# Attention scores of the next tile moved to the end of a step, and one weight buffer shifted by 64 bytes

## The chip, the cores and the metric

The kernel runs on one core of a Trainium2 chip. The metric is the device time of one execution in microseconds, the median of several runs; lower is better.

## The reference

Three computations follow each other. The first is a gated linear-attention recurrence (an mLSTM cell) over 2 batches, 8 heads, 768 time steps and head dimension 40. Its result, 1536 tokens of 320 numbers, goes through an RMS norm and a gated feed-forward layer of width 1536, and then through a second one of width 2048:

```
m' = max(f + m, i);  C = exp(f+m-m')*C + exp(i-m')*outer(v, k);  n = exp(f+m-m')*n + exp(i-m')*k
y  = sigmoid(o) * (C @ q) / max(|n . q|, 1)            # for each head and time step
xn = x / rms(x) * rms_g;   x1 = (silu(xn @ w_gate) * (xn @ w_val)) @ w_out
h  = x1 @ w_in;            out = max(0.01*h, h) @ w_out2
```

## The kernel before, in words

The tokens lie in 12 tiles of 128. For a tile the attention is computed in parallel form: the **scores** (the 8 heads' key-query products, written to PSUM), the product of the scores with a table of decays, the part from the running state (`from_state`), the part from within the tile (`within`), the state's update, a denominator and the output gate (`finish`), the RMS norm, and the **turn**: the normed tile is transposed on TensorE, so that it can be the moving operand of the feed-forward layer. ScalarE and VectorE split what was turned into a high and a low part (`x_high`, `x_low`); every product of the feed-forward layers is made of such parts, at the full rate of the 32-bit round type.

The first feed-forward layer runs in `STEPS1` steps. A step has one block of 128 hidden units and some columns of tokens. The first 20 steps (0 to 19) take two tiles (256 columns, here called **narrow**), those after them four tiles (512 columns, **wide**). In step s TensorE does `gate(s)`, `value(s)` (8 matmuls each) and `out1` of the step before (8 matmuls). The other engines follow: ScalarE takes the tanh of the gate (L606), VectorE multiplies (`gated`, L884, and `hidden1`, L891), ScalarE rounds (`high1`, L620) and VectorE takes the remainder (`low1`, L905). There is one PSUM bank for the gate and one for the value, so `value(s)` waits for `h_done`, which `low1(s-1)` signals, and `gate(s)` waits for `gated(s-1)`.

The attention of tile n runs beside these steps, by a table written out by hand. Its four numbers are the steps after which the pieces come: S (scores), R (from state, within, update), O (denominator, finish) and T (turn). The loops look it up with `work = beside(s - 1)`:

```
BESIDE = {2: (1, 2, 3, 4), 3: (4, 5, 6, 7), 4: (7, 9, 10, 11), 5: (10, 12, 13, 14), 6: (14, 15, 16, 17),
          7: (17, 18, 19, 20), 8: (20, 21, 22, 23), 9: (23, 24, 25, 26), 10: (26, 27, 28, 29),
          11: (29, 30, 31, 32)}
```

Each engine runs its own program in order. TensorE's order in step s is: scores(n) (S) | gate(s) | from_state, within, update_state (R) | value(s) | turn(n) (T) | out1(s-1). `from_state(n)` waits for `p_done`, which VectorE's two products of the scores signal (L784, one for each bank, `scores(n, 0)` and `scores(n, 1)`), and for `x_done`, which `x_low(n-1)` signals. `turn(n)` waits for `xn_done` (ScalarE's L573). `gate` of the first block of a chunk waits for `x_done` of that chunk's last tile. VectorE's order is in the listing. The weights of the first layer (`w1_sb`) lie behind the attention's buffers and a filler (`room`) of which the formula of `used` sets the size.

Of the kernel before, what the change touches and what calls it, by code (L numbers as in the profile page):

```python
# [11 lines left out]
B, H, S, D = 2, 8, 768, 40  # L12
P = 128
DM = H * D
FF1, FF2 = 1536, 2048
SEQ_TILES = S // P
TILES = B * SEQ_TILES
# [24 lines left out]
DV = D + 1  # L42
# [3 lines left out]
PAIRS = H // 2  # L46
# [12 lines left out]
ATT = O0 + DM  # L59
# [22 lines left out]
EXPO = 3  # L82
# [9 lines left out]
def build(nc, first_gates, gates, qk, tok, w1, w2, consts, scratch, out):  # L92
    ctx = ExitStack()
    with ctx:
# [3 lines left out]
        def sb(stack, name, shape, dt=F32):  # L98
            return stack.enter_context(nc.sbuf_tensor(name, shape, dt))
# [21 lines left out]
        with ExitStack() as first:  # L121
            att_sb = sb(first, "att_sb", [P, 2, ATT])

            expo = sb(first, "expo", [P, EXPO, H * P])
            kw = sb(first, "kw", [P, 2, H, D])
            last_decay = sb(first, "last_decay", [P, 2, H])
            num = sb(first, "num", [P, 2, H, DV])


            yt = sb(first, "yt", [P, 2, DM + 1])  # L130
            xn = sb(first, "xn", [P, 2, DM + 1])


            state = sb(first, "state", [P, 2, PAIRS * DV])
            c_tab = sb(first, "c_tab", [P, TILES * H])
            a_tab = sb(first, "a_tab", [P, TILES * H])
            ea_tab = sb(first, "ea_tab", [P, TILES * H])
            dec_tab = sb(first, "dec_tab", [P, TILES * PAIRS])
            den = sb(first, "den", [P, 3 * H])
            ms = sb(first, "ms", [P, 2, 2])  # L140

            unit = sb(first, "unit", [P, P], BF16)
            unseen = sb(first, "unseen", [P, P], BF16)
            used = 4 * (2 * ATT + EXPO * H * P + 2 * H * DV + 6 * DM + 32 + 2 * H + 2 * PAIRS * DV + 3 * TILES * H
                        + TILES * PAIRS + 3 * H + 8) + 4 * P
            if used < 4 * GF * W2:
                sb(first, "room", [P, GF * W2 - used // 4])
            w1_sb = sb(first, "w1_sb", [P, NF1, W1], F32R)
# [19 lines left out]
        def scores_ps(n, z):  # L168

            if n < FIRST:  # L170
                return ((turns[0], gate_ps), (value_ps, out_ps[2]))[n][z]
            return c_ps if z else turns[n % 2]
# [110 lines left out]
        def beside(step):  # L283

            return {piece: [n for n, when in BESIDE.items() if when[i] == step]
                    for i, piece in enumerate("SROT")}
# [13 lines left out]
        def width(s):  # L300
            return STEPS[s][1] * P if s < STEPS1 else CHUNK

        def narrow(s):
            return s < STEPS1 and STEPS[s][1] * P < CHUNK
# [10 lines left out]
        def outs(s):  # L315

            if narrow(s):
                return (s - RING,) if s >= RING else ()
            return (s - RING, s - 1) if narrow(s - 1) else (s - 1,)

        def h_first(s):

            return beside(s - 1)["S"] and beside(s - 1)["O"]
# [403 lines left out]
        def _(dve):  # L727
# [48 lines left out]
            def scores(n, z):  # L776

                dve.wait_ge(s_done, n + 1)


                dve.wait_ge(last_done, n + 1)
                part = expo[:, n % EXPO, :].rearrange("p (q z t) -> p q z t", q=PAIRS, z=2)[:, :, z, :]
                qk_ps = scores_ps(n, z)[:, :].rearrange("p (q t) -> p q t", q=PAIRS)
                nc.vector.tensor_tensor(part, part, qk_ps, ALU.mult).then_inc(p_done, 1)  # L784
# [29 lines left out]
            def denominator(n):  # L814


                dve.wait_ge(pv_done, n + 1)
                both = within_ps(n)[:, 0:H * DV].rearrange("p (h d) -> p h d", h=H)
                if n >= FIRST:
                    dve.wait_ge(inter_used, n - FIRST + 1)  # L820
                    then(nc.vector.tensor_tensor(both, num[:, n % 2, :, :], both, ALU.add))
                nq, other = both[:, :, D:DV], den[:, 2 * H:3 * H].unsqueeze(2)
                then(nc.vector.tensor_scalar(other, nq, -1.0, 1.0, ALU.mult, ALU.max))
                then(nc.vector.scalar_tensor_tensor(out=den[:, 0:H].unsqueeze(2), in0=nq, scalar=1.0, in1=other,
                                                    op0=ALU.max, op1=ALU.max))
                nc.vector.reciprocal(den[:, H:2 * H], den[:, 0:H])
# [131 lines left out]
            low1(0)  # L958
            for s in range(1, STEPS1 + 1):
                work = beside(s - 1)  # L960
                for n in work["S"]:
                    scores(n, 0)
                for n in work["O"]:
                    denominator(n)
                if s < STEPS1:
                    gated(s, width(s))
                if h_first(s):
                    hidden1(s, width(s))
                for n in work["O"]:
                    finish(n)  # L970
                for n in work["S"] if not h_first(s) else ():
                    scores(n, 1)
                for n in work["R"]:
                    from_state(n)
                if s == STEPS1:
                    hidden2(s, s % RING)
                elif not h_first(s):
                    hidden1(s, width(s))
                for n in work["R"]:
                    update_state(n)  # L980
                if s == STEPS1:
                    low2(s, s % RING)
                else:


                    x_first = beside(s)["R"] or s + 1 < STEPS1 and STEPS[s + 1][2] == 0
                    if not x_first:
                        low1(s)
                for n in work["T"]:
                    x_low(n)  # L990
                if s < STEPS1 and x_first:
                    low1(s)
                for n in work["S"] if h_first(s) else ():
                    scores(n, 1)
                if s - 2 in LAST1:
                    x2_odd(LAST1.index(s - 2))
                if s - 1 in LAST1:
                    x2_low(LAST1.index(s - 1))
# [18 lines left out]
            for c in range(CHUNKS - 1):  # L1017
                s = STEPS1 + (CHUNKS + c + 1) * GF
# [8 lines left out]
        def _(pe):  # L1027
# [27 lines left out]
            def scores(n):  # L1055
                pe.wait_ge(qk_in[n % 2], 32 * (n // 2 + 1))
                if n >= FIRST:

                    pe.wait_ge(state_done, n + 1)
                    if n == FIRST:  # L1060
                        pe.wait_ge(y_done, FIRST)
                    else:
                        pe.wait_ge(inter_used, n - FIRST)
                for q in range(PAIRS):
                    pair = slice(q * P, (q + 1) * P)
                    for z in range(2):
                        rows = slice(z * HP, z * HP + D)
                        last = nc.tensor.matmul(scores_ps(n, z)[:, pair],  # L1068
                                                att_sb[rows, n % 2, q * P:(q + 1) * P],
                                                att_sb[rows, n % 2, Q0 + q * P:Q0 + (q + 1) * P],  # L1070
                                                start=True, stop=True)
                last.then_inc(s_done, 1)
# [40 lines left out]
            def turn(n):  # L1113
                pe.wait_ge(xn_done, n + 1)
                if n == 0:

                    pe.wait_ge(tab_done, 2)
                _, x = att_out(n)
                for k in range(2):
                    nc.tensor.transpose(turned_ps(n)[:, k * P:(k + 1) * P], x[:, k * P:(k + 1) * P], ident_sb)  # L1120
                nc.tensor.transpose(odd_ps(n), x[:, 2 * P:DM], ident_sb).then_inc(t_done, 1)
# [128 lines left out]
            value(0)  # L1250
            for s in range(1, STEPS1 + 1):
                work = beside(s - 1)
                for n in work["S"]:
                    scores(n)
                if s < STEPS1:
                    gate(s)
                for n in work["R"]:
                    from_state(n)
                    within(n)
                    update_state(n)  # L1260
                if s < STEPS1:
                    value(s)
                else:
                    in2(s, 0, 0, 0)
                for n in work["T"]:
                    turn(n)
                if s == RING:

                    pe.wait_ge(exp_tab, 2)
                for ready in outs(s):  # L1270
                    out1(ready)
            for g in range(GROUPS):
                for c in range(CHUNKS):
                    for f in range(GF):
                        s = STEPS1 + (g * CHUNKS + c) * GF + f
# [67 lines left out]
```

## Time and profile before

| | |
|---|---|
| median of 3 runs | 442.21 us (441.96 to 442.27) |
| the profiled execution | 442.24 us, span of its instructions 440.5 us |
| TensorE matmuls | busy 428.9 us, 97% of the span |
| VectorE, ScalarE, GpSimd busy | 225.5, 193.8, 92.9 us |
| granted TensorE clock | 1.000 (mean) |

The span is the time from the first instruction to the last. Matmuls overlap, so the time that one takes of the engine is the distance between two starts and not its duration. Narrow steps run from about 21 to 103 us of the span, wide ones to 264 us, and the second layer fills the rest.

### The profile page before, as it was taken

The numbers are of one execution on the slowest core, as the hardware profiler recorded it, in microseconds if no ns is written. First come the engines' busy times: TensorE is split into PE (matmuls) and PEld (weight loads), VectorE is DVE, ScalarE is ACT, GpSimd is POOL, SyncE is SP. The second block draws the span as 40 slices with busy tenths as digits, with TensorE's granted clock in tenths as the row PEclk, the third lists the DMA queues.
The fourth block names the chain that finished last, engine by engine and source line by source line (L and its number), as shares of the span: only waits on it lengthen the run. The fifth ranks groups of instructions, "written<-read, shape, count | busy, mean of one in ns | idle before, by whom it ended". The sixth has DMA issues, their size and how long they took to land.

```text
span 440.5 us, 8225 instructions
## 1 busy us (share of the span) xinstructions
PE 428.9 (97%) x3237; PEld 375.2 (85%) x3237; DVE 225.5 (51%) x435; ACT 193.8 (44%) x431; POOL 92.9 (21%) x98
## 2 busy tenths in 40 slices
PE   6889999999999999999999999999999999999997
PEld 5779998999788888878888888989999999999996
DVE  7656756765466555456433335353333333533534
ACT  4777763655262535234333226553343343333332
POOL 1888862122111111002333003430000000000000
PEclk9999999999999999999999999999999999999999
DMA  6797634331203410001222101400000000100101
GB/s 199 266 309 236 217 110 125 125 111 50 88 18 107 128 49 0 1 1 33 65 67 65 34 1 44 121 1 1 0 1 0 1 1 1 37 25 0 61 0 60
DMA packets 10692, 30.42 MB, mean 69 GB/s; under 512 B 1296, under 2 KB 3264, under 8 KB 10656
## 3 DMA queue, kind: packets, MB, share of 16 engines
q1 hardware_dynamic: 10656, 29.92, 21.1%
q8 instruction: 25, 0.41, 0.4%
q14 instruction: 11, 0.09, 0.1%
HBM read 27.90 MB, written 2.01 MB: 68 GB/s over the span
## 4 chain that ended last, share of the span: by engine, by line
PE 81%; issue 6%; POOL 6%; ACT 3%; DVE 2%; DMA 1%; POOLq 0%; DVEq 0%; ACTq 0%
PE gate_ps L1140 22%; PE value_ps L1140 22%; PE out_ps L1217 9%; PE out_ps L1179 9%; PE turn_ps L1217 6%; POOL w_sb L472 4%; PE out_ps L1183 3%; PE c_ps L1217 3%; PE turn_ps L1107 2%; PE turn_ps L1068 1%; PE turn_ps L1085 1%; ACT expo L543 1%; POOL w_sb L474 1%; POOL expo L441 1%; DMA y_acc<-in_first_gates 1%
## 5 line engine op out<-in xcount | busy, mean ns | idle before, releaser
L1140 PE MATMUL gate_ps<-x_hi,w_sb 128*128 128x512 f32 (+1 forms) x280 | 68.3, 365 | 1.6 <-ACT x_hi L582 0.8
L1140 PE MATMUL value_ps<-x_hi,w_sb 128*128 128x512 f32 (+1 forms) x280 | 68.4, 366 | 1.3 <-DVE h_lo L905 1.3
L1140 PEld LDWEIGHTS gate_ps<-x_hi,w_sb 128*128 128x128 f32 x280 | 46.8, 188 | 10.2 <-issue 1.9
L1140 PEld LDWEIGHTS value_ps<-x_hi,w_sb 128*128 128x128 f32 x280 | 47.1, 188 | 8.7 <-DVE h_lo L905 1.9
L884 DVE SCALAR_TENSOR_TENSOR act_buf<-act_buf,gate_ps 128x512 f32<-128x512 f32 (+1 forms) x46 | 26.2, 569 | 48.0 <-ACT act_buf L606 47.9
L910 DVE TENSOR_TENSOR h_lo<-hid,h_hi 128x512 fp32r<-128x512 f32 x48 | 33.2, 693 | 33.7 <-ACT h_hi L625 33.7
L620 ACT ACTIVATE h_hi<-value_ps 128x512 fp32r<-128x512 f32 (+1 forms) x46 | 23.0, 501 | 59.7 <-DVE value_ps L891 59.5
L1179 PE MATMUL out_ps<-h_hi,w_sb 128*128 128x512 f32 (+1 forms) x184 | 48.2, 348 | 0.0
L625 ACT ACTIVATE h_hi<-hid 128x512 fp32r<-128x512 f32 x48 | 30.3, 632 | 37.6 <-DVE hid L898 36.6
L606 ACT ACTIVATE act_buf<-gate_ps 128x512 f32<-128x512 f32 (+1 forms) x46 | 23.1, 501 | 49.2 <-PE gate_ps L1140 49.1
L480 POOL TENSOR_TENSOR w_sb<-raw,w_sb 128x704 fp32r<-128x704 f32 x16 | 27.6, 1724 | 76.6 <-ACT w_sb L600 76.6
L1217 PE MATMUL out_ps<-w_sb,h_hi 128*128 128x320 f32 x192 | 43.0, 309 | 0.2 <-DVE h_lo L910 0.2
L1140 PE MATMUL gate_ps<-x_lo,w_sb 128*128 128x512 f32 (+1 forms) x140 | 39.1, 360 | 0.0
L1140 PE MATMUL gate_ps<-x_odd,w_sb 128*128 128x512 f32 (+1 forms) x140 | 38.9, 359 | 0.1
L1140 PE MATMUL value_ps<-x_lo,w_sb 128*128 128x512 f32 (+1 forms) x140 | 38.9, 359 | 0.0
L1140 PE MATMUL value_ps<-x_odd,w_sb 128*128 128x512 f32 (+1 forms) x140 | 38.8, 358 | 0.0
L891 DVE SCALAR_TENSOR_TENSOR value_ps<-act_buf,value_ps 128x512 f32<-128x512 f32 (+1 forms) x46 | 26.5, 577 | 21.7 <-PE value_ps L1140 21.4
L905 DVE TENSOR_TENSOR h_lo<-value_ps,h_hi 128x512 fp32r<-128x512 f32 (+1 forms) x46 | 26.5, 575 | 21.1 <-ACT h_hi L620 20.7
L1179 PEld LDWEIGHTS out_ps<-h_hi,w_sb 128*128 128x128 f32 x184 | 31.4, 188 | 3.9
L898 DVE SCALAR_TENSOR_TENSOR hid<-gate_ps,act_buf 128x512 f32<-128x512 f32 x24 | 16.6, 692 | 34.8 <-ACT act_buf L613 34.8
L1217 PEld LDWEIGHTS out_ps<-w_sb,h_hi 128*128 128x128 f32 x192 | 32.7, 188 | 1.8 <-DVE h_lo L910 0.6
L898 DVE SCALAR_TENSOR_TENSOR hid<-value_ps,act_buf 128x512 f32<-128x512 f32 x24 | 16.6, 691 | 30.3 <-ACT act_buf L613 30.3
(150 smaller groups left out, 795.9 us busy)
## 6 DMA issues: line engine op xcount, KB each, us to landing
raw<-in_w SPq DMA_DIRECT2D x12, 544.0 KB, 4.8
att_sb<-in_tok SPq DMA_DIRECT2D x12, 484.0 KB, 4.5
raw<-in_w SPq DMA_DIRECT2D x16, 352.0 KB, 3.0
expo<-decay_scratch SPq DMA_DIRECT2D x10, 512.0 KB, 5.4
att_sb<-in_qk SPq DMA_DIRECT2D x24, 160.0 KB
out_y<-y_acc SPq DMA_DIRECT2D x12, 160.0 KB, 1.9
consts_sb<-in_consts SPq DMA_DIRECT2D x1, 129.5 KB, 2.4
y_acc<-in_first_gates SPq DMA_DIRECT2D x1, 112.0 KB, 2.7
```

Source lines behind the costliest of these rows:

```text
L480: nc.gpsimd.tensor_tensor(w[:, W2RAW:W2], r, w[:, 0:W2RAW].bitcast(F32), ALU.subtract).then_inc(w_lo, 1)
L606: nc.scalar.activation(act_buf[:, s % RING, 0:n], gate_ps[:, 0:n], ACT.Tanh, scale=0.5)\
L620: nc.scalar.activation(h_hi[:, r, cols], value_ps[:, 0:width(s)], ACT.Copy).then_inc(hi_done, 1)
L625: nc.scalar.activation(h_hi[:, r, :], hid[:, r, :], ACT.Copy).then_inc(hi_done, 1)
L884: nc.vector.scalar_tensor_tensor(out=a, in0=a, scalar=1.0, in1=gate_ps[:, 0:n], op0=ALU.add, op1=ALU.mult).then_inc(gate_used, 1)
L891: nc.vector.scalar_tensor_tensor(out=value_ps[:, 0:n], in0=act_buf[:, s % 2, 0:n], scalar=0.5, in1=value_ps[:, 0:n], op0=ALU.mult, op1=ALU ...
L898: nc.vector.scalar_tensor_tensor(out=hid[:, r, :], in0=in_ps[r][:, :], scalar=0.01, in1=act_buf[:, r, :], op0=ALU.mult, op1=ALU.max)\
L905: nc.vector.tensor_tensor(h_lo[:, r, cols], value_ps[:, 0:width(s)], h_hi[:, r, cols].bitcast(F32), ALU.subtract).then_inc(h_done, 1)
L910: nc.vector.tensor_tensor(h_lo[:, r, :], hid[:, r, :], h_hi[:, r, :].bitcast(F32), ALU.subtract).then_inc(h_done, 1)
L1140: last = nc.tensor.matmul(ps[:, 0:n], lhs, rhs, start=(j == 0), stop=(j == len(xs) - 1))
L1179: nc.tensor.matmul(out_ps[k][:, cols], lhs, rhs[:, r, place], start=(f == 0 and t == 0 and j == 0), stop=(f == NF1 - 1 and j == 2))
L1217: ins = nc.tensor.matmul(y_ps(i, k)[:, 0:DM], lhs[:, r, tok], rhs, start=(f == 0 and j == 0), stop=(f == GF - 1 and j == 2))
```

## The change

In a step s in which both a tile's scores and another tile's turn are due (`joined(s)`), TensorE takes the scores behind `value(s)` and `turn`, just ahead of `out1(s-1)`, and no longer ahead of `gate(s)`. VectorE takes both products of the scores at the end of the step, behind `hidden1`, `low1` and `x_low`, and no longer around `gated(s)`. By the table these are the steps s = 5, 8, 15 and 18 (narrow) and 21, 24, 27 and 30 (wide). The scores of tiles 2 and 5 stay where they were. No instruction is added or removed. In the diff the hunks that take `scores(n, 0)` and `scores(n, 1)` are of VectorE's program, those that take `scores(n)` of TensorE's. `room` grows by 64 bytes in each partition, so `w1_sb` begins 64 bytes further on: at 124,864 instead of 124,800 in the partition, the buffers of the second layer's weights and all others staying where they are.

```diff
-            used = 4 * (2 * ATT + EXPO * H * P + 2 * H * DV + 6 * DM + 32 + 2 * H + 2 * PAIRS * DV + 3 * TILES * H
+            used = 4 * (2 * ATT + EXPO * H * P + 2 * H * DV + 6 * DM + 16 + 2 * H + 2 * PAIRS * DV + 3 * TILES * H
...
+        def joined(s):
+            return beside(s - 1)["S"] and beside(s - 1)["T"]
...
-                for n in work["S"]:
+                for n in work["S"] if not joined(s) else ():
                     scores(n, 0)
...
-                for n in work["S"] if not h_first(s) else ():
+                for n in work["S"] if not h_first(s) and not joined(s) else ():
                     scores(n, 1)
...
                 for n in work["S"] if h_first(s) else ():
+                    scores(n, 1)
+                for n in work["S"] if joined(s) else ():
+                    scores(n, 0)
                     scores(n, 1)
...
-                for n in work["S"]:
+                for n in work["S"] if not joined(s) else ():
                     scores(n)
...
                 for n in work["T"]:
                     turn(n)
+                for n in work["S"] if joined(s) else ():
+                    scores(n)
```

## Rows read from the trace of the kernel before

**Rows 1.** The page, part 1: engines, busy us, share, instructions.
```profile
PE 428.9 (97%) x3237; PEld 375.2 (85%) x3237; DVE 225.5 (51%) x435; ACT 193.8 (44%) x431; POOL 92.9 (21%) x98
```

**Rows 2.** Timeline of TensorE around step 18: start, us, engine, line, operation.
```profile
93.34 0.28 PE L1183 MATMUL out_ps<-h_lo,w_sb 128*128 128x256 f32 x1
93.55 0.37 PE L1068 MATMUL turn_ps<-att_sb 40*128 40x128 f32 x1
...
94.64 0.74 PE L1140 MATMUL gate_ps<-x_hi,w_sb 128*128 128x256 f32 x4
...
95.68 0.63 PE L1140 MATMUL value_ps<-x_hi,w_sb 128*128 128x256 f32 x4
...
96.63 0.38 PE L1120 MATMUL turn_ps<-consts_sb,xn 128*128 128x128 f32 x2
...
96.87 0.48 PE L1179 MATMUL out_ps<-h_hi,w_sb 128*128 128x256 f32 x2
...
97.90 0.63 PE L1140 MATMUL gate_ps<-x_hi,w_sb 128*128 128x256 f32 x4
...
99.13 0.68 PE L1085 MATMUL turn_ps<-state,att_sb 40*64 40x41 f32 x32
```

**Rows 3.** Timeline of the other engines around step 18.
```profile
95.03 0.42 DVE L905 TENSOR_TENSOR h_lo<-value_ps,h_hi 128x256 fp32r<-128x256 f32 x1 [0.56 <-ACT h_hi L620]
...
95.37 0.68 DVE L784 TENSOR_TENSOR expo<-expo,turn_ps 128x512 f32<-128x512 f32 x1
95.39 0.57 ACT L573 ACTIVATE xn<-yt,ms 128x320 f32<-128x320 f32 x1 [0.39 <-POOL ms L448]
...
97.16 0.63 ACT L582 ACTIVATE x_hi<-turn_ps,consts_sb 128x128 fp32r<-128x128 f32 x2 [0.89 <-PE turn_ps L1121]
...
98.68 0.34 DVE L871 SCALAR_TENSOR_TENSOR x_odd<-turn_ps,consts_sb,x_odd 64x128 fp32r<-64x128 f32 x1
```

**Rows 4.** Timeline of VectorE: `low1` of the step before, in steps 5, 8 and 15.
```profile
41.66 0.42 DVE L905 TENSOR_TENSOR h_lo<-value_ps,h_hi 128x256 fp32r<-128x256 f32 x1 [0.56 <-ACT h_hi L620]
...
54.13 0.42 DVE L905 TENSOR_TENSOR h_lo<-value_ps,h_hi 128x256 fp32r<-128x256 f32 x1 [0.56 <-ACT h_hi L620]
...
82.60 0.42 DVE L905 TENSOR_TENSOR h_lo<-value_ps,h_hi 128x256 fp32r<-128x256 f32 x1 [0.56 <-ACT h_hi L620]
```

**Rows 5.** Timeline of TensorE: turn of step 5, value of step 9, turn of step 15.
```profile
43.40 0.38 PE L1120 MATMUL turn_ps<-consts_sb,xn 128*128 128x128 f32 x2
...
58.14 0.74 PE L1140 MATMUL value_ps<-x_hi,w_sb 128*128 128x256 f32 x4
...
84.33 0.38 PE L1120 MATMUL turn_ps<-consts_sb,xn 128*128 128x128 f32 x2
```

**Rows 6.** Timeline around the wide step 21 and the head of step 22.
```profile
108.65 0.69 DVE L905 TENSOR_TENSOR h_lo<-value_ps,h_hi 128x512 fp32r<-128x512 f32 x1 [0.67 <-ACT h_hi L620]
...
115.56 0.39 PE L1183 MATMUL out_ps<-h_lo,w_sb 128*128 128x512 f32 x1
...
115.67 0.34 DVE L871 SCALAR_TENSOR_TENSOR x_odd<-turn_ps,consts_sb,x_odd 64x128 fp32r<-64x128 f32 x1
...
116.06 1.20 PE L1140 MATMUL gate_ps<-x_hi,w_sb 128*128 128x512 f32 x4
```

**Rows 7.** Timeline of TensorE: runs of 8 matmuls in step 17, step 41, second layer.
```profile
90.73 0.62 PE L1140 MATMUL gate_ps<-x_hi,w_sb 128*128 128x256 f32 x4
...
91.64 0.62 PE L1140 MATMUL value_ps<-x_hi,w_sb 128*128 128x256 f32 x4
...
235.01 1.07 PE L1140 MATMUL gate_ps<-x_hi,w_sb 128*128 128x512 f32 x4
...
236.84 1.08 PE L1140 MATMUL value_ps<-x_hi,w_sb 128*128 128x512 f32 x4
...
306.24 1.09 PE L1140 MATMUL gate_ps<-x_hi,w_sb 128*128 128x512 f32 x4
...
308.08 0.45 PE L1217 MATMUL out_ps<-w_sb,h_hi 128*128 128x320 f32 x2
```

## The prediction

> **What bounds the kernel now.** I read the page's part 1 first: TensorE's matmuls fill 97% of the span [rows 1]. So I looked for time in two forms only: places where TensorE waits, and work that it does more slowly than it could. For that I went along TensorE's timeline and read distances between starts.
>
> In a narrow step a run of 8 matmuls takes 0.95 us (95.68 to 96.63 [rows 2]). The same run behind the scores takes 1.04 (94.64 to 95.68): starting anew behind small matmuls costs some 0.10. The last matmul ahead of the scores takes 0.21 (93.34 to 93.55) instead of 0.12, another 0.09, and the run behind the turn takes 1.03 (96.87 to 97.90), 0.08 too much. The scores take 1.09 (93.55 to 94.64), the turn 0.24.
>
> The second thing to see is how narrow the cover of `value` is. `value(18)` may start only when `low1(17)` has left the value's bank. That L905 ends at 95.03 + 0.42 = 95.45 [rows 3], and `value(18)` starts at 95.68 [rows 2]. TensorE does not wait, but for 0.23 us only, and because scores and gate (2.13 us) stand ahead of it. L905 is late because VectorE and ScalarE do `finish` and the square of the other tile between `value(17)` and it.
>
> **The change on TensorE, narrow steps (5, 8, 15, 18).** I take step 18 as the pattern.
>
> 1. The gate moves up. It starts at 93.34 + 0.12 = 93.46 and would be done at 94.41.
> 2. `low1(17)` does not move: nothing ahead of it on VectorE, ScalarE or GpSimd changes. It ends at 95.45, and its signal needs some 0.10 (L871 ends at 99.02 [rows 3], the matmul that waits for it starts at 99.13 [rows 2]). So value starts at 95.55. The wait on TensorE is 95.55 - 94.41 = 1.14 us, the place of the scores that had covered it.
> 3. Value takes 0.95 and 0.10 for the new start: turn at 96.60, where it was at 96.63. Its own wait (xn, L573 ends at 95.96 [rows 3]) doesn't bind.
> 4. Then come the scores and out1, where before only out1 came: 96.60 + 0.24 + 0.09 + 1.09 + 0.10 + 0.95 = 99.07 for the head of `gate(19)`, which was at 97.90.
>
> So TensorE loses about what the scores cost, less what it saves in restarts.
>
> **The change on VectorE, steps followed by R.** `from_state` follows one gate later, and it waits for both products of the scores. These were done at 97.32 or earlier, long ahead. Now they are the last things VectorE does in step 18: behind `hidden1`, `x_low` and `low1`. Before, `x_low` ended 99.02 - 96.63 = 2.39 after the turn's start; ScalarE's L582 and VectorE's L871 [rows 3] set that, and it depends on the turn alone. Behind it come now `low1` (0.42) and two products. One ends 0.60 after the operation ahead of it (L784 ends at 96.05, L905 at 95.45 [rows 3]). The matmul starts 2.39 + 0.42 + 1.20 + 0.11 = 4.12 after the turn's start. Before it was 99.13 - 96.63 = 2.50 (then it waited for `x_low` itself). The step loses 1.62 us plus what the turn is late:
>
> - step 18: turn at 96.60 for 96.63, 1.62 - 0.03 = 1.59
> - step 15: L905 ends at 83.02 [rows 4]; turn at 83.02 + 0.10 + 1.05 = 84.17 for 84.33 [rows 5]: 1.46
> - step 5: L905 ends at 42.08 [rows 4]; turn at 43.23 for 43.40 [rows 5]: 1.45. A ScalarE weight copy ahead of xn there (some 0.05) I neglect.
> - step 8 has no R behind it (tile 4's R is a step later). L905 ends at 54.55 [rows 4], turn at 55.70, `gate(9)` at 55.70 + 2.47 = 58.17, `value(9)` at 59.12. Before it stood at 58.14, with a small wait and the 0.10 of a new start (0.74 instead of 0.63 for its four [rows 5]). So it loses 0.88.
>
> The sum is +5.38 us. Nothing behind takes it back that I can find: the steps after are chains that hang on TensorE's own starts, and the weights' copies are ahead of it.
>
> **Wide steps (21, 24, 27, 30).** A run is 1.84 us here. Gate starts about 108.65 and ends at 110.5, and `low1` ends at 109.34 [rows 6], so value doesn't wait. Turn at 112.33; the products are done at 112.33 + 2.39 + 0.69 + 1.20 = 116.6, and `from_state` isn't due before 117.5. So the move costs nothing there, with 0.9 us to spare, and what is left is the saved restarts. Three came with scores and turn before (0.09, 0.10, 0.08), two come now. I take 0.10 a step, between nothing (if turn to scores costs more) and 0.2 (if that change is free): -0.4.
>
> One wait goes away. At the head of step 22 the gate waits for `x_low` of tile 7: 115.56 to 116.06 is 0.50 instead of 0.23, because L871 ends at 116.01 [rows 6]. With the turn 1.3 us earlier that falls: -0.27, and the new start's 0.10 with it, -0.37. Together -0.8.
>
> The order of the small pieces is also what the Trainium skill speaks of: in "TensorEngine Tiling (Array Packing)", Key Properties, it says that a change of the tiling mode drains the engine. By that rule turn next to scores has one change less, as the trace's 0.08 to 0.10 each bear out. Priced by it alone, without the waits, the change would gain, which is the third rival below.
>
> **The 64 bytes.** No row shows this address at work for the first layer. The nearest rows are these. A narrow run takes 0.95 mostly, but in step 17 it takes 0.91 (90.73 to 91.64 [rows 7]), with the same addresses. So there are two paces, which a run seems to pick up at its start. If the shift made all runs quick, 60 narrow runs would give some -2.0 us (0.04 each, about 50 being slow) and, with as much for each of the 78 wide runs, -3.1 more. In the other direction, the second layer, whose weights lie at the same place within 128 bytes as the shifted ones would, takes 1.84 a run where the first takes 1.83 [rows 7]: +0.01 for 78 runs is +0.8. I take nothing, by these last rows, which are the nearest, and keep both ends.
>
> On this the Trainium skill ("TensorE: Matmul & The Clock Gate", Part 2, step 1) says that the engine reads weights and moving data through two ports of its own, so that a load takes nothing from a running matmul. By that an address would change nothing, as I took it; no run yet shows it.
>
> **Sum.** Against the profiled execution's 442.24 us (0.03 above the median of the runs): +5.38 - 0.8 = +4.6, so **446.8 us**.
>
> **Rivals.**
> - *The products are no second wait.* If VectorE gets to them sooner than I have it (say, `x_low` behind them or overlapped), `from_state` starts when the gate is done: turn + 2.47 + 0.95 + 0.12, 0.6 us less in three steps. 4.6 - 1.7 gives 445.1. Against it: the order is written so, and x_low's 2.39 us is a measured chain.
> - *The new address sets the quick pace* in the narrow runs: 446.8 - 2.0 = 444.8; in wide ones too: 441.7, within what counts as no change. For it: the quick pace exists. Against: it comes and goes with one address, and wide runs at either place take the same.
> - *Only restarts count (faster).* With TensorE busy for 97%, the scores may be just work that can stand anywhere, and eight steps each save 0.1 to 0.2, and the wait of 0.37 falls: 442.24 - 1.6 = 440.6. It decides on one place: `low1` of the step before must be done when the gate ends, at 94.4 in step 18. It ended at 95.45, so its chain would have to be 1 us shorter; the scores' absence at the head would have to speed up VectorE's `finish` and `hidden1`, which run ahead of them.
> - *No change that can be told*: losses in narrow and gains in wide steps cancel. That needs the narrow ones to be under 0.2 us each.
>
> **How the numbers follow.** The forecast has 0.60. The first rival has 0.08, the quick narrow runs 0.10, a pace slower by up to 0.01 a run 0.05: all of these are slower than before, 0.83 together. The quick pace everywhere (0.04) and cancelling (0.03) are no change, 0.07. Only restarts: 0.10. What a measurement of this kernel can tell from no change is 0.2%, 0.9 us. The range goes from 443.0, below the quick narrow runs with all restarts saved, to 448.2, the slow pace and 0.2 us more in some narrow steps. The forecast's own range, without a change of pace, is 445.8 to 447.6.
>
> **What would show each step.** In steps 5, 8, 15 and 18 a gap of about 1.1 us ahead of the first value matmul, ended by VectorE's L905, and in steps 6, 16 and 19 one of about 0.6 us ahead of L1085, ended by L784 and not by L871. The granted clock stays 1.00 through these. In steps 21, 24, 27 and 30 no gap, and 0.23 between the last out1 matmul and the gate of step 22. Runs of 8 at 0.95 and 1.83 as now. The span of the wide steps is some 0.8 shorter, that of the narrow ones 5.4 longer. The prediction is wrong if L905 ends early enough, if the products are done before the gate, or if the pace of the long runs of wide steps moves in the second digit.

## The result, and the profile after

The changed kernel takes 447.50 us (median of 4 runs, 446.79 to 447.86), the one before 442.24 (441.96 to 442.61): 5.3 us more, a ratio of 1.0118 with a 95% interval of 1.0103 to 1.0133. The forecast was 446.8. The profiled executions stand at 447.86 and 442.24, their spans at 446.1 and 440.5.

The page, part 1, hides it: the instructions are the same, and TensorE is busy for the same share as before [rows 1].

```profile
PE 430.7 (97%) x3237; PEld 377.8 (85%) x3237; DVE 225.5 (51%) x435; ACT 193.1 (43%) x431; POOL 92.4 (21%) x98
```

In the waits of the changed kernel (engine and line, who released it: us in total, times, longest), two stand out. L909 is `low1` there, L788 the product of the scores, L1147 the gate and value, L1092 `from_state`.

```profile
PE value_ps L1147 <- DVE h_lo L909: 5.0, 7, 0.8
PE turn_ps L1092 <- DVE expo L788: 1.5, 3, 0.5
```

Before, the first of them came to 1.3 us in two places, at 26.51 and 30.52, far ahead of the steps that changed, and the second wasn't there:

```profile
PE value_ps L1140 <- DVE h_lo L905: 1.3, 2, 0.7
```

The timeline of the changed kernel around step 18 answers to [rows 2, 3]:

```profile
98.15 0.64 PE L1147 MATMUL gate_ps<-x_hi,w_sb 128*128 128x256 f32 x4
...
99.52 0.42 DVE L909 TENSOR_TENSOR h_lo<-value_ps,h_hi 128x256 fp32r<-128x256 f32 x1 [0.56 <-ACT h_hi L624]
...
100.00 0.74 PE L1147 MATMUL value_ps<-x_hi,w_sb 128*128 128x256 f32 x4 [0.72 <-DVE h_lo L909]
...
101.06 0.38 PE L1127 MATMUL turn_ps<-consts_sb,xn 128*128 128x128 f32 x2
101.27 0.27 PE L1128 MATMUL turn_ps<-consts_sb,xn 128*64 128x128 f32 x1
...
101.47 0.37 PE L1075 MATMUL turn_ps<-att_sb 40*128 40x128 f32 x1
...
103.48 0.42 DVE L909 TENSOR_TENSOR h_lo<-value_ps,h_hi 128x256 fp32r<-128x256 f32 x1
...
103.63 0.64 PE L1147 MATMUL gate_ps<-x_hi,w_sb 128*128 128x256 f32 x4
103.83 0.68 DVE L788 TENSOR_TENSOR expo<-expo,turn_ps 128x512 f32<-128x512 f32 x1
...
104.42 0.68 DVE L788 TENSOR_TENSOR expo<-expo,c_ps 128x512 f32<-128x512 f32 x1
...
105.25 0.38 PE L1092 MATMUL turn_ps<-state,att_sb 40*64 40x41 f32 x11 [0.50 <-DVE expo L788]
```

The gate starts at 98.15 and would be done some 0.96 later, at 99.11. Value starts at 100.00, right behind L909's end at 99.94: TensorE stands for 0.9 us. At the other end, `from_state` starts at 105.25, behind the second L788, which ends at 105.10. Both waits are where the prediction put them, and the steps lose within 0.15 us of what it said. From the head of a step (its first matmul, be it of the scores or of the gate) to the head of the one two later, steps 5 and 6 take 1.52 us more than before, 8 and 9 0.99, 15 and 16 1.61, 18 and 19 1.53.

One wait was not foreseen. It is in the wide step 24:

```profile
135.00 1.12 PE L1147 MATMUL gate_ps<-x_hi,w_sb 128*128 128x512 f32 x4
...
137.06 0.69 DVE L909 TENSOR_TENSOR h_lo<-value_ps,h_hi 128x512 fp32r<-128x512 f32 x1 [0.66 <-ACT h_hi L624]
...
137.81 1.20 PE L1147 MATMUL value_ps<-x_hi,w_sb 128*128 128x512 f32 x4 [0.78 <-DVE h_lo L909]
```

Gate to value is 2.81 us there and 1.81 in step 27. And the paces have moved (a pace is the time from one matmul's start to the next one's). From the gate of step 35 to that of step 45 the changed kernel takes 54.40 us (10 steps of 24 matmuls, 0.2267 each). Before, by the same two gates, it was 202.05 to 256.99: 54.94, 0.2289 each.

```profile
208.33 1.07 PE L1147 MATMUL gate_ps<-x_hi,w_sb 128*128 128x512 f32 x4
...
262.73 1.07 PE L1147 MATMUL gate_ps<-x_hi,w_sb 128*128 128x512 f32 x4
```

The mean distance of two starts in a run of narrow matmuls went the other way, from 0.1171 to 0.1196 us.

### The profile page after: what moved, and what is told of

It reads as the page before. It is cut to its first block, busy times and chain, and to the rows that moved or that the text cites. A ratio compares the mean times of both kernels' runs of the same rounds, so it can differ in the third digit from the quotient of the medians.

```text
span 446.1 us, 8225 instructions
## 1 busy us (share of the span) xinstructions
PE 430.7 (97%) x3237; PEld 377.8 (85%) x3237; DVE 225.5 (51%) x435; ACT 193.1 (43%) x431; POOL 92.4 (21%) x98
## 4 chain that ended last, share of the span: by engine, by line
PE 75%; issue 8%; POOL 6%; DVE 5%; ACT 4%; DMA 1%; DVEq 0%; POOLq 0%; ACTq 0%
PE value_ps L1147 21%; PE gate_ps L1147 20%; PE out_ps L1224 9%; PE out_ps L1186 8%; PE turn_ps L1224 6%; POOL w_sb L476 4%; PE c_ps L1224 3%; PE out_ps L1190 3%; PE turn_ps L1114 2%; ACT expo L547 2%; PE turn_ps L1092 1%; PE turn_ps L1075 1%; DVE value_ps L895 1%; DVE expo L788 1%; POOL w_sb L478 1%
## 5 line engine op out<-in xcount | busy, mean ns | idle before, releaser
L1147 PE MATMUL value_ps<-x_hi,w_sb 128*128 128x512 f32 (+1 forms) x280 | 69.1, 369 | 5.0 <-DVE h_lo L909 5.0
L1147 PE MATMUL gate_ps<-x_hi,w_sb 128*128 128x512 f32 (+1 forms) x280 | 67.8, 364 | 0.9 <-ACT x_hi L586 0.8
L1147 PEld LDWEIGHTS value_ps<-x_hi,w_sb 128*128 128x128 f32 x280 | 47.5, 190 | 13.3 <-DVE h_lo L909 6.7
L1147 PEld LDWEIGHTS gate_ps<-x_hi,w_sb 128*128 128x128 f32 x280 | 47.8, 191 | 8.2 <-issue 1.2
L1147 PE MATMUL gate_ps<-x_lo,w_sb 128*128 128x512 f32 (+1 forms) x140 | 39.2, 362 | 0.0
L1147 PE MATMUL value_ps<-x_lo,w_sb 128*128 128x512 f32 (+1 forms) x140 | 39.2, 362 | 0.0
L1147 PE MATMUL value_ps<-x_odd,w_sb 128*128 128x512 f32 (+1 forms) x140 | 39.1, 361 | 0.0
L1147 PE MATMUL gate_ps<-x_odd,w_sb 128*128 128x512 f32 (+1 forms) x140 | 39.0, 361 | 0.0
L909 DVE TENSOR_TENSOR h_lo<-value_ps,h_hi 128x512 fp32r<-128x512 f32 (+1 forms) x46 | 26.5, 575 | 20.9 <-ACT h_hi L624 20.7
```

The costliest lines, as they stand in the source:

```text
L909: nc.vector.tensor_tensor(h_lo[:, r, cols], value_ps[:, 0:width(s)], h_hi[:, r, cols].bitcast(F32), ALU.subtract).then_inc(h_done, 1)
L1147: last = nc.tensor.matmul(ps[:, 0:n], lhs, rhs, start=(j == 0), stop=(j == len(xs) - 1))
```

## The experiments

Each was timed beside the kernel before on the same chip. The head of step 5 lies between 39.49 and 40.72 us in the 14 traces, and between 39.87 and 40.71 in the six that have the same work and the same address ahead of it, so traces are compared from there on.

**The two parts alone.** The first keeps `joined` and the new orders and sets the filler back, the second has nothing but the filler:

```diff
 e1: changed kernel with
-... + 6 * DM + 16 + 2 * H ...
+... + 6 * DM + 32 + 2 * H ...
 e2: kernel before with
-... + 6 * DM + 32 + 2 * H ...
+... + 6 * DM + 16 + 2 * H ...
```

> The move of the scores without the 64 bytes. My theory now: in the changed kernel the move costs about 6.9 us (narrow steps 5, 8, 15, 18 and the ones behind them 5.7, step 24 1.2), and the new address takes about 0.055 us off each of the 26 wide steps (-1.4) and adds about 0.01 to 0.02 for each run of 8 narrow matmuls (+1). So this kernel should be at +5.3 to +6 us against before, with runs of 8 at 0.94 and 1.83 us as in the kernel before. Rival (the paces follow the order of the work, not the address): +5.3 us too, but runs of 8 at 0.96 and 1.81 as in the changed kernel.

> The 64 bytes without the move. If the address sets the pace: runs of 8 narrow matmuls at 0.96 instead of 0.94 (+1.2 us), wide ones at 1.81 instead of 1.83 (-1.4 us), together within 0.5 us of before, and a trace in which narrow steps are longer and wide steps shorter. Rival (the address does nothing, as two read ports of their own would have it): paces as before and the time too.

The move alone took 447.88 us against 442.07: +5.8, ratio 1.0129 (1.0113 to 1.0144). Its paces are those of before, 0.2289 wide and 0.1175 narrow. The shift alone took 441.59: -0.5, ratio 0.9988 (0.9979 to 0.9997), with 0.2267 and 0.1196, those of the changed kernel. So the paces follow the address and not the order of the work. In the trace of the move alone the step pairs lose 1.57, 1.01, 1.64 and 1.57 us, and get 0.25 back in the steps ahead of them (no new start at the scores): 5.5 us.

**The wide steps.** Both are the move alone (e1) with a narrower condition:

```diff
-            return beside(s - 1)["S"] and beside(s - 1)["T"]
+            return beside(s - 1)["S"] and beside(s - 1)["T"] and s in (21, 27, 30)      # e3
+            return beside(s - 1)["S"] and beside(s - 1)["T"] and s == 24                # e4
```

> The move in the wide steps 21, 27 and 30 alone, address as before. My forecast's step for these: restarts saved 0.1 each and the wait at step 22 gone (-0.37): -0.7 us. What the changed kernel's trace says: turn to scores costs 0.17 and not 0.09, so nothing is saved in restarts, and -0.3 to -0.4 us is left. Rival (PE-bound, only restarts count): -1.0 us.

> The move in step 24 alone, address as before. In step 24 value waits for the low part of step 23, which is late because VectorE and ScalarE split the output of the first chunk (x2) ahead of it; the scores had covered that. My forecast had taken this step as free. Expected now: +1.1 us (0.9 of wait and 0.1 to 0.2 for the new start). If the wait in the changed kernel's trace was a thing of its narrow steps' delay or of the address: 0.

Steps 21, 27 and 30 alone gave 441.54 us against 442.07: -0.5, ratio 0.9987 (0.9978 to 0.9996). Nearly all of it is at the head of step 22: steps 20 to 22 take 0.39 us less, steps 26 and 27 the same together as before (5.49 + 7.13 for 5.58 + 7.04). Step 24 alone gave 443.18: +1.1, ratio 1.0026 (1.0016 to 1.0037), with the same wait as in the changed kernel though nothing is late ahead of it:

```profile
129.53 1.09 PE L1147 MATMUL gate_ps<-x_hi,w_sb 128*128 128x512 f32 x4
...
132.27 1.21 PE L1147 MATMUL value_ps<-x_hi,w_sb 128*128 128x512 f32 x4 [0.73 <-DVE h_lo L909]
```

**Is it the cover that counts?** Here the scores stand in the same eight steps behind the gate, with VectorE's order of before:

```diff
-                for n in work["S"]:
+                for n in work["S"] if not work["T"] else ():
                     scores(n)
                 if s < STEPS1:
                     gate(s)
+                for n in work["S"] if work["T"] else ():
+                    scores(n)
```

> Scores behind the gate and ahead of the value in the same eight steps, VectorE's order and the address as before. If the loss in the narrow steps is the bare wait of value for the low part of the step before, the scores cover it from this place as well: value starts within 0.1 us of where it did, and the time is that of before (-0.3 to +0.5 us). Rival (what costs is that gate and scores part from the head of the step, that is the order of the banks or of the restarts): +2 us or more.

441.87 us against 441.96, ratio 1.0000 (0.9990 to 1.0009). In step 18 value starts 2.13 us after the step's head, as it did in the kernel before (93.55 to 95.68 [rows 2]), and no wait for L905 is in the profile:

```profile
93.14 0.63 PE L1140 MATMUL gate_ps<-x_hi,w_sb 128*128 128x256 f32 x4
...
94.18 0.37 PE L1068 MATMUL turn_ps<-att_sb 40*128 40x128 f32 x1
...
95.27 0.74 PE L1140 MATMUL value_ps<-x_hi,w_sb 128*128 128x256 f32 x4
```

So the scores hide the wait from either place ahead of value; behind value they hide nothing. This kernel also has VectorE's order of before, so it doesn't tell the two waits apart: the next two runs do.

**The second wait.** e1, with the products between `x_low` and `low1` in the steps followed by R:

```diff
+                early = joined(s) and x_first
+                for n in work["S"] if early else ():
+                    scores(n, 0)
+                    scores(n, 1)
                 if s < STEPS1 and x_first:
                     low1(s)
...
-                for n in work["S"] if joined(s) else ():
+                for n in work["S"] if joined(s) and not early else ():
```

> The move without the 64 bytes, and in the steps followed by R VectorE takes both products of the scores ahead of the low part and no longer behind it. If they are the second wait, the state's products start about 0.4 us sooner in steps 6, 16 and 19: 1.2 us less than the move alone, +4.6 us against before. Rival (the state's part waits for something else, such as the low part of x, which ends 1.7 us before): as the move alone, +5.8 us.

447.17 us against 441.96: +5.2, ratio 1.0114 (1.0096 to 1.0132), 0.6 less than the move alone by the medians, where 1.2 was expected. In the trace steps 5 to 19 take 67.38 us (to the head of step 20) where e1 takes 68.40: 1.0 less. In steps 6, 16 and 19 `from_state` starts 1.30 us after the gate and no longer 1.64. The products still come last, but only a little later than the gate is done:

```profile
103.29 0.68 DVE L788 TENSOR_TENSOR expo<-expo,c_ps 128x512 f32<-128x512 f32 x1
103.89 0.42 DVE L909 TENSOR_TENSOR h_lo<-value_ps,h_hi 128x256 fp32r<-128x256 f32 x1
...
104.12 0.68 PE L1096 MATMUL turn_ps<-state,att_sb 40*64 40x41 f32 x32 [0.20 <-DVE expo L788]
```

**The first wait, made shorter.** e1, with `hidden1` and the rounding ahead of `finish` and the square in the steps before the narrow ones:

```diff
-            return beside(s - 1)["S"] and beside(s - 1)["O"]
+            return beside(s - 1)["O"] and (beside(s - 1)["S"] or s + 1 in (5, 8, 15, 18))
```

> The move without the 64 bytes, and in the steps ahead of the narrow ones (4, 7, 14, 17) VectorE takes hidden1 ahead of finish and ScalarE the rounding ahead of the square. My account says that value waits for the low part because finish and the square stand ahead of it: then the low part comes about 0.6 us sooner and the wait of value falls to 0.4 us. The normed tile comes later by about 0.4 in exchange, so that the turn waits for it: 0.2 to 0.5 us less a step than the move alone, +4 to +5 us against before. Rival (value waits for something that these do not move): as the move alone, +5.8 us, the wait at 0.9 still.

448.06 us against 441.95: +6.1, ratio 1.0142 (1.0126 to 1.0157), no gain over the move alone, where +4 to +5 was expected. The mechanism holds: value of step 18 comes 1.52 us after its gate and not 1.92 as in e1, and in steps 5, 8 and 15 some 1.37 and not 1.90. But the normed tile is late by more than I took, and the turn waits for it, which eats the gain:

```profile
PE turn_ps L1127 <- ACT xn L577: 1.9, 5, 0.5
```

**Where the weights lie.** Four more places for `w1_sb` in the kernel before, by the number in the formula of `used` alone (24, 48, 80 and 64 for 32):

> The kernel before with the first layer's weights 32 bytes further on. At 0 from a multiple of 128 bytes a narrow matmul took 117.1 ns and a wide one 229.1, at 64 from it 119.6 and 227.5. If the pace follows the distance from such a multiple, this place at 32 may give a third pair of paces; if only the half of 128 matters, the first pair.

> The kernel before with the first layer's weights 64 bytes back, so that they lie at 64 from a multiple of 128 bytes as in the changed kernel, but 128 bytes from there. If the place within 128 bytes sets the pace, it is that of the changed kernel: 119.6 and 227.5 ns, time -0.5 us against before. If it is the absolute address (or what else lies there): any other pair.

> The kernel before with the first layer's weights 192 bytes back. Four places gave four pairs of paces, and none follows the place within 128 bytes. All of a block's weights keep their place within 256 bytes, and the moving data (x and h) lie at 192 from a multiple of 256. If that place sets the pace, this address, at 192 as in the changed kernel, gives the changed kernel's pair: 119.6 ns narrow and 227.4 wide, and the time -0.5 us. Rival (the absolute address): another pair again, as the 64 bytes back gave with 118.6 and 232.3.

> The kernel before with the first layer's weights 128 bytes back, at 0 from a multiple of 256 bytes. The runs so far say that the place within 256 bytes sets the pace: 192 gave 0.2267 us for a wide matmul at two addresses, 128 gave 0.2289, 64 gave 0.2324 and 160 gave 0.2333. If the pace is best where the weights lie like the moving data (192) and falls off to either side, 0 gives one like 128, 0.229, and the time is within 0.3 us of before. If only the distance to the moving data in one direction counts, 0 may be as slow as 64: +2 us.

Within a partition, all pieces of the weight blocks keep their place within 256 bytes, since every offset into them is a multiple of that. `x_hi`, `x_lo`, `x_odd`, `h_hi` and `h_lo` lie at 192 in it. Wide is the distance of the gates of steps 35 and 45 by 240, narrow the mean distance of starts in runs of narrow matmuls. The kernels with the address of before lie between 0.117 and 0.118 in the narrow pace, so 0.1171 and 0.1173 can't be told apart; their wide pace is 0.2289 in every trace. Each ratio is against the kernel before as it was timed beside that run.

| weights moved by | place in 256 bytes | narrow, us | wide, us | time against before, ratio (95%) |
|---|---|---|---|---|
| -192 | 192 | 0.1196 | 0.2267 | 0.9988 (0.9978 to 0.9998) |
| -128 | 0 | 0.1147 | 0.2333 | 1.0033 (1.0022 to 1.0044) |
| -64 | 64 | 0.1186 | 0.2324 | 1.0061 (1.0043 to 1.0079) |
| 0 (before) | 128 | 0.1171 | 0.2289 | 1 |
| +32 | 160 | 0.1173 | 0.2333 | 1.0050 (1.0032 to 1.0068) |
| +64 (the change) | 192 | 0.1196 | 0.2267 | 0.9988 (0.9979 to 0.9997) |

My first thought, that 128 bytes matter, fell with -64, which shares that place with +64 and is 2.45 us slower than before. The second, 256 bytes, was tested with -192 and held: another address, the same pair of paces as +64. The last guess, that 0 would be as good as 128 for the wide ones, fell (0.2333), while its narrow runs are the quickest of all. The wide pace at -192 is read from the same two gates:

```profile
202.25 1.07 PE L1140 MATMUL gate_ps<-x_hi,w_sb 128*128 128x512 f32 x4
...
256.65 1.07 PE L1140 MATMUL gate_ps<-x_hi,w_sb 128*128 128x512 f32 x4
```

**The two gains together.** e3 with the 64 bytes:

> The move in steps 21, 27 and 30 alone, with the 64 bytes: the two parts that each took 0.5 us off. They touch different things (a wait at the head of step 22, the pace of the runs), so they should add: -1.0 us against before, 441.1 us. Rival (one part's gain hangs on the other): -0.5 us.

440.82 us against 441.95: -1.1, ratio 0.9972 (0.9962 to 0.9983). They add, and this kernel is quicker than both the one before and the changed one.

## Why the prediction was right

- **Gate up, value waits** (narrow steps, points 1 to 4): held, with a smaller wait. It is 0.9 us in step 18 and not 1.14: `low1` ends 1.79 us after the gate's start, where I had it at 1.99 (95.45 - 93.46). The turn comes 1.06 after value, as worked out (0.95 and 0.10), and the scores start 0.09 later behind the turn than I took, which makes up for part of it. That the missing cover is the cause is shown from two sides: with the scores ahead of value the loss is gone (e5), and with a sooner `low1` value starts sooner (e9).
- **The products as second wait**: held. From the turn to `from_state` it is 105.25 - 101.06 = 4.19 us, worked out as 4.12. e6 took the two products ahead of `low1` and got 1.0 us back in the trace of these steps, 0.6 by the medians. So the rival without a second wait fell.
- **Their sum**, +5.38: the move alone lost 5.5 in steps 4 to 19.
- **Wide steps**: the term of the sum that failed. I worked out step 21 and wrote that "the move costs nothing there" for all four. In step 24 the low part comes at 137.75, 2.75 after the gate's start, where step 21 had it at 0.7, and that costs 1.1 us (e4). The trace suggests why: the first chunk ends with step 21, and behind it both engines split that chunk's output (`x2`) ahead of their usual work. On VectorE this stands between `low1(22)`, which starts at 129.38, and the denominator at 133.19:

```profile
131.39 1.29 DVE L921 TENSOR_TENSOR x_lo<-out_ps,x_hi 128x512 fp32r<-128x512 f32 x2 [1.32 <-ACT x_hi L635]
132.59 0.67 DVE L924 TENSOR_TENSOR tail<-out_ps,tail 64x512 f32<-64x512 f32 x1
```

  From the start of that `low1` to the end of `finish` it is 6.42 us, and 4.43 at the same place three steps later, where nothing is split. The low part is late by the same 2.0 us. No run took this work away. The wide steps must be read one by one.
- **Saved restarts**, -0.4: not there. I had taken turn to scores at 0.09 like out1 to scores. In the trace it is 101.27 to 101.47, 0.20 where the turn's last matmul had been followed after 0.03 (96.84 to 96.87), so 0.17 more. Scores and turn cost 0.27 in new starts before, and about the same now (0.17 and 0.10). The Trainium skill's rule that a change of the tiling mode drains the engine ("TensorEngine Tiling (Array Packing)", Key Properties) agrees with these traces in that each change costs something, but counting the changes would have given a gain that isn't there: they don't cost the same.
- **The wait at the head of step 22**, -0.37: held (0.39 less in steps 20 to 22 of e3).
- **The 64 bytes**, taken as nothing: -0.5 us in the whole kernel (e2), and not the same everywhere. By the steps of the two traces e2 takes 0.56 us more than the kernel before from the head of step 5 to that of step 20, and 0.95 less from there to that of step 45. So the rival of a new pace was half true: the wide runs are quicker, the narrow ones slower. My argument from the second layer's runs (1.84 for 1.83) compared unlike things. By the listing the second layer's weights lie at 192 within 256 bytes in every run; there a run stands behind matmuls of another form, and in the kernel before too its first five distances between starts are 0.228 to 0.235 us and only the last two 0.227. The Trainium skill ("TensorE: Matmul & The Clock Gate", Part 2, step 1) says that loading weights takes no read bandwidth from a running matmul. I had concluded from it that the address could change nothing, and e2, e7, e8, e11 and e12 show that it does; the measurement decides. Whether the weights' load or something else is slower isn't shown.
- **The signs that I had named against it**: two came up. Value waits in step 24, and the wide runs of 8 moved in the second digit, from 1.83 to 1.81. Between the heads the changed kernel's steps 5 to 19 are 5.7 us longer (5.4 forecast), and its steps 20 to 44 0.4 shorter (0.8 forecast).

The sum with what was measured: 5.5 + 1.1 - 0.4 = 6.2 for the move, where the medians say 5.8, less 0.5 for the address: 5.3 to 5.7. The forecast of 4.6 is 0.7 short. That it came so close is in part luck: a missed wait (+1.1) and a saving that isn't there (+0.4) were partly balanced by the address (-0.5). The rival of restarts alone (440.6) fell at the place it named: `low1` was not done when the gate ended.

## What to carry to other kernels

A busy engine may do small work just ahead of an instruction that needs the result of a long chain on other engines. That work may hide the chain's lateness, and moved behind the instruction it becomes pure cost, even with the engine at 97%. So look at how soon after its release an instruction starts, and not only at the waits that exist. Read every instance of a pattern, above all the ones at a chunk's border. And when buffers move, however little, time both parts alone.

## What the runs showed of the hardware that I had not expected

The pace of back-to-back matmuls with a fresh weight load each depends on the weights' address, and by these runs on its place within 256 bytes: 0.2267 to 0.2333 us for 512 columns (3%) and 0.1147 to 0.1196 for 256 columns (4%), and the place that is best for the one is the worst for the other. The period of 256 bytes rests on one pair of addresses, 256 bytes apart, that gave the same two paces to 0.0001 us. Whether it is the place itself or the distance to the moving data (at 192 in all runs) was not tried: no kernel moved `x` or `h`. What in the memory or the array makes it so stays open.
